# A batch's exponentials and its attention weights swap roles on TensorE: the product comes out with keys on partitions

## The reference

```python
k_p = k.reshape(B, H, Sp, 8, D).mean(axis=3); v_p = v.reshape(B, H, Sp, 8, D).mean(axis=3)
scores = scale * (q @ k_p.T);  attn = exp(scores - max);  attn = attn / (attn.sum(-1) + 1e-9)
x = (attn @ v_p), heads side by side              # 4608 tokens x 512
logits = x @ phi                                  # 4608 x 32
d = np.exp(logits - logits.max(0)); d /= d.sum(0, keepdims=True) + 1e-9
slot_input = (d.T @ x).reshape(E, S_per_e, D)     # sums over all 4608 tokens
for e in range(E): slot_out[e] = np.maximum(slot_input[e] @ w1[e], 0.0) @ w2[e]
c = softmax of logits over the slots;  y = c @ slot_out
out = (s * np.maximum(y @ w_in, 0)**2 + b) @ w_out
```

## Time and profile before

| | before |
|---|---|
| median of 3 runs | 681.06 us (680.16 to 683.78) |
| the profiled execution | 680.44 us, of which the span of the profile is 678.6 us |
| TensorE matmul busy | 647.3 us (95%) |
| VectorE / ScalarE / GpSimd busy | 371.8 / 326.4 / 114.8 us |
| granted TensorE clock, mean | 0.986 |

### The profile page before, as it was taken

One profiled execution on the slowest core, in us unless ns is written; L12 is line 12 of the kernel. 1 busy time (PEld: TensorE's weight loads), 2 busy tenths in 40 slices (PEclk: granted clock), 3 DMA queues, 4 the chain that ended last, 5 costly groups with the idle time before them and its releaser, 6 DMA issues.

```text
span 678.6 us, 13190 instructions
## 1 busy us (share of the span) xinstructions
PE 647.3 (95%) x5170; PEld 504.5 (74%) x5170; DVE 371.8 (55%) x619; ACT 326.4 (48%) x607; POOL 114.8 (17%) x117
## 2 busy tenths in 40 slices
PE   7788999999988889999999999999999999999997
PEld 6566777767743248888888888888888888888885
DVE  5757675656344646764454455554554545545543
ACT  1577777777411265554344443443444434443442
POOL 3899787622110000000000000000000000000000
PEclk9799999999998989999999999999999999999999
DMA  9688969563679920010010010000000100100101
GB/s 340 222 265 312 350 245 377 177 271 127 228 290 430 427 114 1 1 60 3 1 63 1 1 62 0 30 32 0 31 31 0 62 0 0 62 1 0 63 0 63
DMA packets 25233, 80.45 MB, mean 119 GB/s; under 512 B 6496, under 2 KB 14688, under 8 KB 22368
## 3 DMA queue, kind: packets, MB, share of 16 engines
q1 hardware_dynamic: 25184, 79.76, 31.5%
HBM read 70.32 MB, written 9.44 MB: 118 GB/s over the span
## 4 chain that ended last, share of the span: by engine, by line
PE 82%; DMA 7%; POOL 5%; issue 2%; DVE 2%; ACT 1%; ACTq 0%; SPq 0%; DVEq 0%; POOLq 0%
PE bank L1459 19%; PE bank L1461 19%; PE bank L1460 19%; PE bank L1443 5%; DMA late<-in_moe_w_dram 4%; PE bank L1311 4%; POOL kvbuf L657 2%; PE bank L1298 2%; DMA kvbuf<-in_k_dram 2%; PE bank L1235 2%; PE bank L1268 2%; PE bank L1393 2%; PE bank L1340 1%; PE bank L1356 1%; POOL kvbuf L664 1%
## 5 line engine op out<-in xcount | busy, mean ns | idle before, releaser
L1459 PE MATMUL bank<-w_hi,r_hi 128*128 128x512 f32 x576 | 224.2, 389 | 1.4 <-DVE r_lo L1092 1.4
L1460 PE MATMUL bank<-w_lo,r_hi 128*128 128x512 f32 x576 | 224.1, 389 | 0.0
L1461 PE MATMUL bank<-w_hi,r_lo 128*128 128x512 f32 x576 | 224.1, 389 | 0.0
L1086 DVE SCALAR_TENSOR_TENSOR win_sb<-win_sb,sb_col 128x512 f32<-128x512 f32 x144 | 108.5, 753 | 197.5 <-ACT win_sb L839 197.5
L839 ACT ACTIVATE win_sb<-bank 128x512 f32<-128x512 f32 x144 | 86.1, 598 | 217.8 <-PE bank L1443 217.8
L1459 PEld LDWEIGHTS bank<-w_hi,r_hi 128*128 128x128 f32 x576 | 108.1, 188 | 24.4 <-DVE r_lo L1092 2.0
L1461 PEld LDWEIGHTS bank<-w_hi,r_lo 128*128 128x128 f32 x576 | 108.1, 188 | 22.4
L1460 PEld LDWEIGHTS bank<-w_lo,r_hi 128*128 128x128 f32 x576 | 108.1, 188 | 22.4
L1092 DVE SCALAR_TENSOR_TENSOR r_lo<-win_sb,sb_col,r_hi 128x512 fp32r<-128x512 f32 x144 | 107.6, 747 | 1.5 <-ACT r_hi L848 1.5
L848 ACT ACTIVATE r_hi<-win_sb,sb_col 128x512 fp32r<-128x512 f32 x144 | 103.2, 717 | 1.6 <-PE bank L1461 1.6
L1443 PE MATMUL bank<-cT,g_st 128*128 (+1 forms) x144 | 56.4, 393 | 0.0
(11 more groups left out here) (133 smaller groups left out, 560.6 us busy)
## 6 DMA issues: line engine op xcount, KB each, us to landing
early_third<-in_moe_w_dram SPq DMA_DIRECT2D x6, 2048.0 KB, 14.2
kvbuf<-in_k_dram SPq DMA_DIRECT2D x12, 768.0 KB, 5.6
kvbuf<-in_v_dram SPq DMA_DIRECT2D x12, 768.0 KB, 5.9
out_dram<-win_sb SPq DMA_DIRECT2D x36, 256.0 KB, 2.4
qbuf<-in_q_dram SPq DMA_DIRECT2D x8, 1024.0 KB, 8.0
early<-in_moe_w_dram SPq DMA_DIRECT2D x4, 2048.0 KB, 12.4
late<-in_moe_w_dram SPq DMA_DIRECT2D x4, 2048.0 KB, 20.1
win_sb<-in_moe_w_in_dram SPq DMA_DIRECT2D x4, 1024.0 KB, 5.3
```

Source lines behind the costliest of these rows:

```text
L1086: dve.scalar_tensor_tensor(out=g_sb[:, n % 2, :], in0=r_sb[:, n % 2, :], scalar=sb_col[:, 0:1], in1=r_sb[:, n % 2, :], op0=ALU.mult, op1=A ...
L1459: pe.matmul(acc, r2_hi[:, f % 2, toks], w_hi[:, f, :], start=(f == 0), stop=False)
L1460: pe.matmul(acc, r2_hi[:, f % 2, toks], w_lo[:, f, :], start=False, stop=False)
L1461: last = pe.matmul(acc, r2_lo[:, f % 2, toks], w_hi[:, f, :], start=False, stop=(f == F2C - 1))
```

## The change

- The product takes the weights of one head as the stationary operand (128 x 73) and the exponentials of a tile (32 columns) as the moving one: for each head four matmuls and one for the mixed unit, added up in PSUM. So a half has 20 matmuls, and a batch 40. The result has keys (and the 73rd lane) on partitions and the tiles already added.
- `b_sb`, its two copies, the eight matmuls against `fold` and their step are gone. ScalarE copies the result to `bT` in one piece of 73 x 256 (for the last batch in two pieces of 73 x 128). The sums come one step earlier.
- The denominator is made by four matmuls of 73 x 32 against one column of the identity, in place of one of 128 x 128.
- `dl` has the mixed tile beside the four others, so one subtraction and one exponential of 128 x 160 take the place of two each.
- At the end the sums of the last batch are added straight into `sum_n`; the division by the denominator moves behind the first experts' product, as a scale of the copy at line 810. GpSimd clears `hT` after `sT` is written.

```diff
-        b_sb = sb("b_sb", [P, 2, DEN], where=att)
-        bT = sb("bT", [KEYS, H, SLOTS], where=att)
+        bT = sb("bT", [LANES, H, SLOTS], where=att)
...
-        def bT_step(g):
+        def sums_step(g):
             return b_step(g, 1) + 1
-
-        def sums_step(g):
-            return b_step(g, 1) + 2
...
+        def b_bank(g, half):
+            return bank[S_B[0] if g == B - 1 and half else B_B]
+
+        def b_col(g, h):
+            return SLOTS * (h % HB if g == B - 1 else h)
...
-            pool.wait_ge(ps_ready, B)
+            pool.wait_ge(sT_kept, 1)
...
-                    rows = slice(HALF * (g % 2), HALF * (g % 2 + 1))
                     act.wait_ge(misc_read, misc_reads("row", g))
-                    act.wait_ge(dl_ready, g + 1)
-                    act.activation(dl[:, g % 2, 0:QT, :], dl[:, g % 2, 0:QT, :], ACT.Exp).then_inc(d_ready, 1)
-                    act.activation(dl[rows, g % 2, QT, :], dl[rows, g % 2, QT, :], ACT.Exp).then_inc(d_ready, 1)
+                    act.activation(dl[:, g % 2, :, :], dl[:, g % 2, :, :], ACT.Exp).then_inc(d_ready, 1)
...
-                for g, half in b_halves(n - 1):
-                    act.wait_ge(b_ready, 2 * g + half + 1)
-                    if g:
-                        act.wait_ge(ps_ready, g)
-                    act.activation(b_sb[:, half, :], b_bank(g, half)[:, 0:DEN], ACT.Copy).then_inc(b_kept, 1)
-                for g in groups_with(bT_step, n - 1):
-                    act.wait_ge(bT_ready, g + 1)
-                    if g:
-                        act.wait_ge(ps_ready, g)
-                    act.activation(bT[:, :, :], bank[B_B][0:KEYS, 0:H * SLOTS].rearrange("k (h s) -> k h s", s=SLOTS),
-                                   ACT.Copy).then_inc(bT_kept, 1)
+                for g in groups_with(sums_step, n):
+
+                    pieces = 1 if g < B - 1 else 2
+                    for x in range(pieces):
+                        heads = H // pieces
+                        act.wait_ge(b_ready, 2 * g + 2 // pieces * (x + 1))
+                        if g:
+                            act.wait_ge(ps_ready, g)
+                        act.activation(bT[:, heads * x:heads * (x + 1), :],
+                                       b_bank(g, x)[0:LANES, 0:heads * SLOTS].rearrange("k (h s) -> k h s", s=SLOTS), ACT.Copy).then_inc(bT_kept, 1)
...
+                    act.wait_ge(den_ready, 1)
                     rows = BANK // F1C
                     for half in range(2):
                         act.activation(h_sb.rearrange("p (c q) -> p c q", c=F1C)[:, :, rows * half:rows * (half + 1)],
-                                       bank[2 + half][:, :].rearrange("p (q c) -> p c q", c=F1C), ACT.Copy).then_inc(h_kept, 1)
+                                       bank[2 + half][:, :].rearrange("p (q c) -> p c q", c=F1C), ACT.Copy,
+                                       scale=over_den[:, 1:2]).then_inc(h_kept, 1)
                 act.wait_ge(cT_psum, n + 1)
                 act.activation(turned(n, slice(0, P)), turn_bank(n, slice(0, P)), ACT.Copy).then_inc(cT_hi, 1)
...
-                    dve.tensor_tensor(dl[:, g % 2, 0:QT, :], logits[:, first:first + QT, :], row.unsqueeze(1).to_broadcast([P, QT, SLOTS]),
-                                      ALU.subtract).then_inc(dl_ready, 1)
-                    dve.tensor_tensor(dl[rows, g % 2, QT, :], logits[rows, mixed, :], row[rows], ALU.subtract).then_inc(misc_read, 1)
+                    dve.tensor_tensor(dl[:, g % 2, :, :], logits[:, group_tiles(g), :], row.unsqueeze(1).to_broadcast([P, QT + 1, SLOTS]),
+                                      ALU.subtract).then_inc(misc_read, 1)
...
+                    if g == B - 1:
+
+                        dve.wait_ge(ps_kept, g)
+                        dve.wait_ge(fall_kept, g)
+                        dve.scalar_tensor_tensor(out=sum_n[:, :, :], in0=sums[:, 0:P].rearrange("p (x c) -> p c x", c=DC),
+                                                 scalar=falls[:, g:g + 1], in1=bank[B_B][:, 0:P].rearrange("p (x c) -> p c x", c=DC),
+                                                 op0=ALU.mult, op1=ALU.add).then_inc(last_step, 1)
...
-            dve.wait_ge(ps_kept, B)
-            dve.tensor_scalar(over_den[:, 0:1], sums[:, P:P + 1], float(1.0 / np.float32(EPS)), EPS, ALU.mult, ALU.add).then_inc(last_step, 1)
             dve.wait_ge(last_step, 1)
-            dve.reciprocal(over_den[:, 1:2], over_den[:, 0:1]).then_inc(last_step, 1)
+            dve.transpose(sum_t[:, :, :].rearrange("p c s -> p (c s)"), sum_n[:, :, :].rearrange("p c x -> p (c x)")).then_inc(last_step, 1)
             dve.wait_ge(last_step, 2)
-            dve.tensor_scalar(sum_n[:, :, :], sums[:, 0:P].rearrange("p (x c) -> p c x", c=DC), over_den[:, 1:2], None,
-                              ALU.mult).then_inc(last_step, 1)
-            dve.wait_ge(last_step, 3)
-            dve.transpose(sum_t[:, :, :].rearrange("p c s -> p (c s)"), sum_n[:, :, :].rearrange("p c x -> p (c x)")).then_inc(last_step, 1)
-            dve.wait_ge(last_step, 4)
             dve.wait_ge(sT_zero, 1)
             dve.tensor_copy(own_slots(sT, DC), sum_t[:, :, :].rearrange("p c (e s) -> p c e s", e=EXPERTS)).then_inc(sT_kept, 1)
+
+            dve.scalar_tensor_tensor(out=over_den[:, 0:1], in0=sums[:, P:P + 1], scalar=falls[:, B - 1:B], in1=bank[B_B][:, P:P + 1],
+                                     op0=ALU.mult, op1=ALU.add).then_inc(last_step, 1)
+            dve.wait_ge(last_step, 3)
+            dve.tensor_scalar(over_den[:, 0:1], over_den[:, 0:1], float(1.0 / np.float32(EPS)), EPS, ALU.mult, ALU.add).then_inc(last_step, 1)
+            dve.wait_ge(last_step, 4)
+            dve.reciprocal(over_den[:, 1:2], over_den[:, 0:1]).then_inc(den_ready, 1)
...
-                    found = b_bank(g, half)
+                    rows = slice(HALF * (g % 2), HALF * (g % 2 + 1))
                     keep_warm(n, half == 0)
-                    pe.wait_ge(d_ready, 2 * (g + 1))
-                    if g == B - 1:
+                    pe.wait_ge(d_ready, g + 1)
+                    if half == 0:
+                        pe.wait_ge(ps_kept, g) if g else pe.wait_ge(vn_kept, 2)
+                    elif g == B - 1:
                         pe.wait_ge(sx_ready, UNITS)
-                    elif half:
-                        pe.wait_ge(b_kept, 2 * g + 1)
-                    else:
-                        pe.wait_ge(ps_kept, g) if g else pe.wait_ge(vn_kept, 2)
-                    for j in range(QT):
-                        rhs = ex[:, units[j] % EXR, HB * (j % 2):HB * (j % 2 + 1), :].rearrange("p a k -> p (a k)")
-                        pe.matmul(found[QUAD * j:QUAD * (j + 1), 0:DEN], dl[:, g % 2, j, :], rhs,
-                                  start=True, stop=False, skip_group_check=True)
                     for a in range(HB):
-
-                        lanes = LANES if a == 0 else KEYS
-                        last = pe.matmul(found[QUAD * a:QUAD * (a + 1), LANES * a:LANES * a + lanes], dl[:, g % 2, QT, :],
-                                         ex[:, mixed % EXR, HB * (a % 2) + (HB * half + a) // 2, 0:lanes],
+                        h = HB * half + a
+                        found = b_bank(g, half)[0:LANES, b_col(g, h):b_col(g, h) + SLOTS]
+                        for j in range(QT):
+                            pe.matmul(found, ex[:, units[j] % EXR, HB * (j % 2) + a, :], dl[:, g % 2, tile_of(g, j), :],
+                                      start=(b_col(g, h) == 0 and j == 0), stop=False, skip_group_check=True)
+                    for a in range(HB):
+                        h = HB * half + a
+                        found = b_bank(g, half)[0:LANES, b_col(g, h):b_col(g, h) + SLOTS]
+                        last = pe.matmul(found, ex[rows, mixed % EXR, HB * (h % 2) + h // 2, :], dl[rows, g % 2, mixed_of(g), :],
                                          start=False, stop=True, skip_group_check=True)
                     last.then_inc(b_ready, 1)
-                for g in groups_with(bT_step, n):
-                    keep_warm(n, 1)
-                    pe.wait_ge(b_kept, 2 * g + 2)
-                    if g:
-                        pe.wait_ge(ps_kept, g)
-                    for h in range(H):
-                        x = h % HB
-                        last = pe.matmul(bank[B_B][0:KEYS, SLOTS * h:SLOTS * (h + 1)], b_sb[:, h // HB, LANES * x:LANES * x + KEYS],
-                                         fold[:, 0, :], start=True, stop=True)
-                    last.then_inc(bT_ready, 1)
                 for g in groups_with(sums_step, n):
 
                     i, bb = g // 2, g % 2
                     keep_warm(n, 1)
-                    pe.wait_ge(bT_kept, g + 1)
+                    pe.wait_ge(bT_kept, g + 1 if g < B - 1 else B + 1)
                     pe.wait_ge(vn_kept, 2 * (i + 1))
-                    pe.matmul(bank[B_B][:, P:P + 1], fold[:, :, :].rearrange("p a s -> p (a s)"), b_sb[:, 0, KEYS:LANES],
```

(18 more changed lines are left out.)

14 lines of the change are left out of this document (3 added, 11 removed).

## The result

| | before | after |
|---|---|---|
| median | 681.23 us (680.16 to 683.78, 4 runs) | 715.81 us (712.06 to 716.96, 4 runs) |
| profiled execution, its span | 680.44, 678.6 us | 716.96, 715.2 us |
| granted TensorE clock, mean | 0.986 | 0.969 |

The ratio is 1.050 [1.046, 1.053]: the kernel is 34.6 us slower, where +20.4 was forecast, and 6.8 us above the range's upper end. The new page has more records and more load time than the earlier trace rows; the second line is the clock in 40 slices.

A forecast was written before the change was run, and what follows sets the result against it. TensorE's program order was taken as the bound up to 180 us, then a chain of waits and the DMA stream of matrices. Terms of 16.2 + 2.8 + 3.85 - 2.2 gave +20.6 us, predicted 701.5 us, range 690 to 709.

The forecast's parts named there:

- The price of the product: Attention's new product: 80 load records a batch, paced by the load at 66 ns, 5.28 us a batch.
- I give them the same 66 ns: Mixed unit's 16 records a batch, 64 rows each: assumed at 66 ns like full ones, lower bound 44 ns.
- 2.64 a half: Half a batch's new product on TensorE: 2.64 us, against 0.76 us for the old half.
- Attention, batches 0 to 5: First six batches: even ones +3.0 us each, odd ones +2.4, together +16.2 us.
- Batches 6 and 7: End of attention: last product starts 2.8 us later than 187.02 from this stretch, and itself takes 5.28 us, +3.85.
- Pauses of TensorE without a cause in the profile: Unexplained TensorE stops, listed in the forecast's own range: may come or go by 1 or 2 us.
- The tail: From last product to experts: 3.3 us of chain gone, but only the DMA engines' 2.2 us gap can be won.
- The sum: Whole kernel: 22.85 - 2.2 = +20.6 us; 701.0 on the profiled execution, 701.7 on the median.
- (a): Rival on the product: loads hide and the stream sets the pace, 27 ns a record; 677.5 us, chance 4%.
- (b): Rival on attention: extra work fills waiting the windows don't show, batches 0 to 5 cost nothing; 685.5 us, chance 8%.
- (c): Rival on the product: loads and streams don't overlap, 94 ns a record; 718 us, chance 6%.
- The signs: Trace if right: 1280 load records 60 to 70 ns apart, last product 20 to 23 us later, squared ReLU layer unchanged.

The follow-up runs named there:

- the later matrices: The changed kernel with only the sixth and seventh expert matrix issued after the ninth: 710.65 us, ratio 1.046.
- 64 columns: The changed kernel with each product matmul streaming 64 columns instead of 32, in all batches, loads unchanged: 706.47 us, ratio 1.039.
- both costs away: The changed kernel with 64 columns streamed in the product and the sixth and seventh expert matrix issued after the ninth: 702.79 us, ratio 1.032.
- 64 columns in the last two batches: The changed kernel streaming 64 columns per product matmul in batches 6 and 7 only, 32 in the others: 705.78 us, ratio 1.040.
- all matrices late: The changed kernel with all nine expert matrices loaded after the last scores: 724.54 us.
- tail-alone run: The kernel before with only the change's end: sums straight into sum_n, division as a scale of line 810, hT cleared later: 679.79 us, ratio 0.9996.

## Why the prediction was right or wrong

The miss of 14.3 us adds up in two orders, all from medians of different rounds: after to the later matrices -5.2, from there to 64 columns as well -7.9 (710.65 to 702.79), rest +1.3; or 64 columns first -9.3, then the matrices -3.7, rest +1.3. Some of it is shared, since a pause is dearer when the clock sinks behind it. The profiled executions give it by stage, 716.96 against the 701.0 forecast: batch 6's product starts 8.2 us later than forecast (205.36 against 180.99 + 16.2), the way from there to the last product is 3.7 longer, the last product 5.2, the tail 0.5, and 1.4 comes off in the experts, for a reason given below. That is 16.2 of 16.0.

- **The price of the product: right in mechanism and in pace, under-sized as a term.** 66 ns a record was measured, for the mixed records too, so "I give them the same 66 ns" holds; half the rows makes a load no shorter. What "2.64 a half" left out are the changes of group, 0.12 us each, on top of the pace: into the mixed records and out of them. The old half was measured to the start of the next group (0.76) and has its way out in it, the new one hadn't. A half is 2.91 instead of 2.64 us, 4.3 us over 16 halves.
- **Attention, batches 0 to 5: right.** +15.2 us without the pauses against +16.2. Since the halves were 12 x 0.27 = 3.2 us dearer than forecast, other steps were 4.2 us cheaper, and the agreement to 1 us is partly luck. Some 2.4 of these would be pauses of the kernel before itself, 1.45 at 145.95 and 0.90 at 90.69, which have no like there; the rest I can't place.
- **Batches 6 and 7: this step failed.** Last product to start at 206.0: with both costs away 207.74, after 217.86. It was to take 5.28 us: 5.9 with both away (the changes of group again), 10.5 after. The step took its pace from rows at the granted clock 1.00 and never asked whether the new work would keep it. Clock at the end: 8.0 us from after to 64 columns in the last two batches (61.5 against 69.4, above), 9.6 us with the matrices moved (70.5 against 60.9, same stretch); the medians give 7.9 to 10.0.
- **Pauses: named, but far under-sized; this step failed too.** "Pauses of TensorE without a cause in the profile may come or go by 1 or 2 us" was short for each of the two alone, in the profiled execution. Between the same two halves of the product it took 22.80 us over the pause at 106 (94.07 to 116.87) and 18.68 with all matrices late, 22.05 over the one at 158 and 17.6 with two or all of them late: 4.1 and 4.4 us, low clock included. The long ones did have a sign in the profile: the DMA engines are full beside them (share 1.01 at 143 to 146 before, 1.09 and 0.99 at the two places of after). The one of 0.90 stands beside idle DMA engines (0.05), so transfers aren't the whole cause. Full DMA engines don't always bring a stop either: the earlier trace rows has them at 1.02 with none.
- **The tail: right.** -2.2 us forecast. From the end of the last product to the end of the experts' second product it was 236.7 - 188.5 = 48.2 us before, 45.5 with both costs away (259.1 - 213.6), and 46.5 after. There is no gap of the DMA engines in the former (share 0.95 and more from 217 to 221 us), as forecast. After there is one again at 236, since the half clock delays line 1385's first weights:

```profile
236.00:237.00 1.00, 1.00 (x12) 0.24 (x8) 0.93 (x3) 0.00 (x0) 0.00 (x0) 1.00 0.21 82
```

- **The sum** was made against an execution that had its own mishap. There, line 1430's first group took 3.34 us; in the tail-alone run and after, the same group takes 1.92: the 1.4 us above. The clock in the kernel before at that place was:

```profile
239.00:240.00 1.00, 1.00 (x8) 0.22 (x4) 0.00 (x0) 0.00 (x0) 0.00 (x0) 0.58 0.96 410
240.00:241.00 1.00, 1.00 (x8) 0.22 (x4) 0.00 (x0) 0.53 (x1) 0.00 (x0) 0.50 1.11 475
```

- **The rivals.** (a) would have needed under 45 ns a record, and 66 was measured; (b) needed hidden waiting, and attention grew by what the halves cost; (c) gave 718 (its own terms add up to about 719) and so came nearest in total, by another mechanism: 66 instead of 94 ns, and the stream doubled for nothing. A total that fits doesn't prove its rival; the pace of one burst decided.
- **The signs.** "Some 1280 load records" was a slip: 8 batches of 80 are 640, and 640 are there; the sum itself went by 80 a batch. 60 to 70 ns apart: yes, 66. The last product 20 to 23 us later: its start is 20.7 later without the two costs, 30.8 with them. The squared ReLU layer as long as before: yes.

## What to carry to other kernels

Price a float32 matmul with a narrow moving operand by its load, from a row of the same shape, take the changes between groups of different rows in as well (0.12 us each here), and remember that here the streamed columns were free up to 64. Ask of every stretch that the change fills with such matmuls whether it keeps the clock at which the price was read: among transposes and scores it held, where they stood almost alone it fell to half and nearly doubled their price. Read the baseline's own pauses and low-clock windows before summing against its profile, and ask which transfers run beside the work that grows. A stop without a semaphore is worth setting against the packets of the instruction queue.

## What the runs showed of the hardware

- TensorE had next to no idle time from 205 us on, and yet its granted clock went from 1.00 to 0.50 and stayed there for some 24 us. Streaming 64 instead of 32 columns under the same loads kept it at 1.00 for no time of its own. In the five microseconds before the fall the load row was as busy as in the kernel that kept the clock (4.62 of 5 us against 4.51), so that row doesn't foretell it. What exactly the chip measures these runs don't show. The Trainium skill (TensorE: Matmul & The Clock Gate, section LDWEIGHTS) gives a load as columns over 1.2 per ns, 0.83 a column; the trace agrees in the slope (0.8 to 0.9) and has about 5 ns more on each record (66 instead of 61 for 73 columns).
- TensorE stopped for up to 2.8 us in the middle of bursts without a semaphore. The stops stand at places a multiple of 256 of its records apart and end 1.2 to 1.6 us after a 16 KB packet of the instruction queue has landed. The ones of 1.4 us and more stood beside full DMA engines (share 0.9 and more); with two or more transfers moved, five kernels had none at 155, but one of them had one at 120 instead. The stop at 106 us came (1.55) in the kernel with the two transfers moved and didn't come when 64 columns were streamed (its packet then came 8 us behind the one before, in place of 11.5). What decides when a packet is fetched these runs don't show. With all matrices late a wait of about 1 us for VectorE's logits is left there.
- A change from loads of 128 rows to loads of 64 rows cost time. Between 73-column loads, 66 ns apart, the first 64-row one came 187 ns behind the last 128-row one. 32-column matmuls of 64 rows right behind ones of 128 rows waited 0.47 us each time.
